# The first 64 rows of the last two experts in one shared fp32 tile ahead of the expert loop

## The chip, the cores and the metric

The kernel runs on one core of one Trainium2 chip. What counts is device time in microseconds (us), from the start to the end of one launch.

## The reference

Three stages follow each other. Attention with a mask that keeps the 32 largest scores of each row (4 batches, 8 heads, 576 rows, head size 64) gives x of 2304 x 512. A dense layer with a squared ReLU, `(relu(x @ w_in)**2) @ w_out` with 2048 hidden columns, gives the next x. Then each row goes to one of eight experts, or to none:

```python
do_compute = x @ w_skip > 0
out = x.copy()
xc = x[do_compute]
logits = xc @ w_gate
e_idx = np.argmax(logits, axis=1)
gate_w = softmax(logits)[np.arange(len(xc)), e_idx]
for e in range(8):
    mask = e_idx == e
    h = np.maximum(xc[mask] @ w1[e], 0.0)      # w1[e]: 512 x 1024
    y[mask] = gate_w[mask, None] * (h @ w2[e]) # w2[e]: 1024 x 512
out[do_compute] = xc + y
```

With the inputs used here 921 of the 2304 rows are kept: 244, 93, 269, 118, 84, 48, 48 and 17 for experts 0 to 7.

## The kernel before

All engines run one written-out program each, and semaphores order them. The first 750 us are the attention and the dense layer, interleaved in a loop over time steps `t` (to `TIMES`); TensorE is busy nearly without a gap. The rows of x are worked in nine groups of 256 (`ORDER`); the last group's two column blocks are called late, the sixteen before it early.

The router is worked out by VectorE in many short dependent operations on tiles of 2 to 18 columns per partition (`link` makes each wait for the one before it): which expert each row has (`pick_experts`), its gate (`set_gates`), its rank within its expert (`my_rank`), how many 128-row tiles each expert needs (`ntiles`) and where they begin (`tile_from`), and from these the tile (`my_tile`) and place of each row. TensorE turns this into a table of row numbers by 18 small matmuls (L1565); from it VectorE sets `gather_tab` (L1240), and GpSimd gathers the rows of a tile from `rows_gated` in DRAM by an indirect DMA (L739).

To cover this wait, one tile is worked ahead: the first 128 early rows of expert 0 (`ahead_rows`, `ahead_w1`, `ahead_w2`), in plain fp32 with the raw weights. Its up matmuls (`up_ahead`, L1481), its transposes (`transpose_ahead`) and its down matmuls (L1586) are placed among the table's steps on TensorE. Six of the eight down matmuls come before the transposes of tile 0's rows (`transpose_rows(0)`, L1573), which wait for the gather, and two after.

The expert loop then runs over tiles `s`, each with one expert, in the order of experts. Each tile is computed to nearly fp32 accuracy from fp32r products of high and low parts: ScalarE writes the high part of each weight piece (`w1_high` L966, `w2_high` L972), VectorE and GpSimd the low part (`w1_low` L1267, `w2_low` L1273 and L735), and TensorE multiplies high by high, low by high and high by low (L1600, L1605, L1609 up; L1631, L1636, L1639 down). The w1 pieces of tile `s + 1` are split in the second half of tile `s`; two of VectorE's four are made before the result `yo` of tile `s` (L1300), which GpSimd scatters to `out` (L763). The first four tiles always run, the rest under `If(tiles > s)`.

Raw weights lie in `weights`, three slots of 32 KB per partition (w1 in the first half, w2 in the second). The loop uses slots 0 and 1 in turn by the expert's number; slot 2 is the place of `w1_high` and `w2_high`. Before, slots 1 and 2 held the split `w_in` of the dense layer. SyncE loads each expert in four pieces of 1 MB (`load_expert`, L474), two outstanding; an expert's load starts when the splits of the expert two before it are done. All eight experts are loaded whatever the counts, and SyncE waits for all of them at the end, reads four registers and waits for the scatters. Which slot and which load a tile needs is read from `meta` into registers; past the last tile the tables name expert 7.

Of the kernel before, what the change touches and what calls it, by code (L numbers as in the profile page):

```python
# [52 lines left out]
def build(nc, qT, kT, v_main, v_tail, w_in, w_out, w9, w1, w2, rows_scratch, out):  # L53
# [74 lines left out]
    MIDDLE = N // 2  # L128
    E = NE
# [10 lines left out]
    with ExitStack() as ctx:  # L140
# [53 lines left out]
        with (nc.sbuf_tensor("values", [P, NCOL, 2, SLOTS], F16) as values,  # L194
              nc.sbuf_tensor("ahead_rows", [P, D + 4], F32) as ahead_rows, nc.sbuf_tensor("ahead_xT", [P, D], F32) as ahead_xT,
              nc.sbuf_tensor("ahead_values", [P, EARLY, 2], F16) as ahead_values):
            pass
# [118 lines left out]
        ahead_stored = sem("ahead_stored")  # L316
        places_set = sem("places_set")
# [26 lines left out]
        ahead_w2 = weights[:, 0, KC * F2:WCOL].rearrange("p (f n) -> p f n", f=F2T)  # L344
        xg = tail[:, 3 * F2:3 * F2 + DEEP * (D + 4)].rearrange("p (b n) -> p b n", b=DEEP)
# [22 lines left out]
        expert, parity, empty = (temp(SLOTS) for _ in range(3))  # L368
        ahead = temp(EARLY)
# [63 lines left out]
        def _(sp):  # L433
# [48 lines left out]

            load_kq(0)
# [13 lines left out]
            for t in range(TIMES):  # L497
# [43 lines left out]
                for j in range(GROUPS):  # L541
                    if ENDS[j] != t:
                        continue
                    sp.wait_ge(rows_copied, 2 * j + (2 if j < GROUPS - 1 else 1))
# [13 lines left out]

            for e in range(1, E):
                if e == 1:  # L560

                    sp.wait_ge(unit_up, NU)
# [7 lines left out]
                for n in range(4):  # L570
# [3 lines left out]
                    if e >= RING and n == 2:  # L574

                        wait_apart(sp, w2_low_v, 3 * first + 1)
                        wait_apart(sp, w2_low_p, first + 1)
                    if e == 1 and n == 2:

                        sp.wait_ge(gates_set, 2)  # L580
                        store_gates(ORDER[-1][0] * S + ORDER[-1][1] * W, [EARLY, EARLY + 1])
                    load_expert(e, n)
            for par in range(2):
                sp.wait_ge(expert_loaded[par], 2 * E * LOADS)
            sp.wait_ge(ahead_stored, 16)
            turns = [sp.value_load(meta[0:1, x:x + 1], min_val=1, max_val=TURNS)
# [5 lines left out]
        def _(pool):  # L592
# [144 lines left out]
            def gather(s):  # L737
# [5 lines left out]

            gather(0)
# [10 lines left out]
                in_=yo[:, DEEP - 1, :], in_offset=None, bounds_check=N - 1, oob_is_err=False).then_inc(ahead_stored, 16)  # L755

# [20 lines left out]
        def _(act):  # L777
# [173 lines left out]
            exponentiate_logits(EARLY, 2)  # L951
            rectify_ahead(0)
            rectify_ahead(1)
            copy_ahead(0)
            copy_ahead(1)
            act.wait_ge(meta_set, 1)
# [24 lines left out]
            def routed_tile(s):  # L981
# [4 lines left out]
                wait(act, down_done, s)  # L986
                split_w2_high(at, (3, 0, 1))
                place[:] = [expert_at(act, s + 1), expert_need(act, s + 1)]
                act.wait_ge(up_done, 2 * s + 1)
                if s == 0:  # L990

                    act.wait_ge(ahead_down, 1)
# [173 lines left out]


# [521 lines left out]
```

## Time and profile before

| | us |
|---|---|
| median of 3 runs | 924.42 (924.35 to 924.54) |
| the profiled execution | 924.49 |
| its span, first to last instruction | 922.7 |
| TensorE (PE) busy in it | 883.8 |
| VectorE (DVE) busy | 819.3 |
| ScalarE (ACT) busy | 658.5 |
| GpSimd (POOL) busy | 656.9 |

The span is counted from the first instruction; some 1.8 us of the execution lie around it. Times in the rows below are from the span's start. Busy shares are means over stages that differ; the change acts on the last 170 us, so those have to be read by themselves.

### The profile page before, as it was taken

The numbers are of one execution on the slowest core, as the hardware profiler recorded it, in microseconds if no ns is written. First come the engines' busy times: TensorE is split into PE (matmuls) and PEld (weight loads), VectorE is DVE, ScalarE is ACT, GpSimd is POOL, SyncE is SP. The second block draws the span as 40 slices with busy tenths as digits, with TensorE's granted clock in tenths as the row PEclk, the third lists the DMA queues.
The fourth block names the chain that finished last, engine by engine and source line by source line (L and its number), as shares of the span: only waits on it lengthen the run. The fifth ranks groups of instructions, "written<-read, shape, count | busy, mean of one in ns | idle before, by whom it ended". The sixth has DMA issues, their size and how long they took to land.

```text
span 922.7 us, 21066 instructions
## 1 busy us (share of the span) xinstructions
PE 883.8 (96%) x6674; PEld 716.9 (78%) x6674; DVE 819.3 (89%) x2584; ACT 658.5 (71%) x1297; POOL 656.9 (71%) x884
## 2 busy tenths in 40 slices
PE   3799899999999999999999999999999999999997
PEld 1677688887888878888788887888878886788886
DVE  5999999999999999999999999999992064888887
ACT  2778787777777778777777777877775322788886
POOL 1899998877877887787787788778777552444432
PEclk9999999999999999999999999999999999999999
DMA  8963543466343658956545455543533775764990
GB/s 307 361 235 97 185 142 124 139 213 195 134 165 129 207 185 273 257 177 231 167 141 164 136 178 178 175 124 118 187 122 117 243 249 203 266 235 149 348 336 10
DMA packets 69750, 175.40 MB, mean 190 GB/s; under 512 B 21298, under 2 KB 26418, under 8 KB 65280
## 3 DMA queue, kind: packets, MB, share of 16 engines
q1 hardware_dynamic: 67792, 168.91, 54.8%
q0 software_dynamic: 1840, 5.06, 1.8%
q8 instruction: 56, 0.92, 0.4%
q14 instruction: 62, 0.51, 0.2%
HBM read 154.19 MB, written 21.27 MB: 190 GB/s over the span
## 4 chain that ended last, share of the span: by engine, by line
PE 84%; DVE 11%; POOL 2%; issue 1%; ACT 1%; DMA 0%; SPq 0%; DVEq 0%; POOLq 0%
PE psum L1334 8%; PE psum L1399 7%; PE psum L1400 7%; PE psum L1401 7%; PE psum L1359 7%; PE psum L1416 7%; PE psum L1417 7%; PE psum L1378 7%; PE psum L1418 7%; DVE top L1036 3%; DVE upper L1041 3%; PE psum L1631 2%; PE psum L1600 2%; PE psum L1605 2%; PE psum L1636 2%; PE psum L1639 2%
## 5 line engine op out<-in xcount | busy, mean ns | idle before, releaser
L1036 DVE MAX8 top<-upper 128x8 f32<-128x288 f32 x576 | 239.0, 446 | 0.0
L620 POOL TENSOR_TENSOR s_sb<-s_sb,below 128x576 f32<-128x576 f32 x144 | 203.3, 1433 | 1.5 <-ACT below L792 1.5
L1041 DVE MATCH_REPLACE8 upper<-top,upper 128x288 f32<-128x288 f32 x432 | 187.7, 441 | 0.0
L1399 PE MATMUL psum<-x_high,w_in_high 128*128 128x256 f32 x576 | 168.2, 292 | 1.6 <-POOL x_low L626 1.1
L783 ACT ACTIVATE s_sb<-psum 128x576 f32<-128x576 f32 x144 | 93.8, 651 | 96.9 <-PE psum L1334 87.4
L1400 PE MATMUL psum<-x_low,w_in_high 128*128 128x256 f32 x576 | 161.8, 281 | 0.0
L1401 PE MATMUL psum<-x_high,w_in_low 128*128 128x256 f32 x576 | 161.2, 280 | 0.0
L635 POOL TENSOR_TENSOR square<-relu 128x256 f32<-128x256 f32 x144 | 89.6, 622 | 81.6 <-ACT relu L825 80.9
L640 POOL TENSOR_TENSOR g_low<-square,g_high 128x256 fp32r<-128x256 f32 x144 | 108.4, 753 | 30.2 <-POOL square L635 23.0
L1334 PE MATMUL psum<-k_sb,q_sb 64*128 64x288 f32 x512 | 101.3, 473 | 26.8 <-DVE lower L1027 18.6
L792 ACT ACTIVATE below<-s_sb,steep_kth 128x576 f32<-128x576 f32 x144 | 110.8, 770 | 9.3 <-POOL neg_max L608 8.4
L1051 DVE MAX8 top<-lower 128x8 f32<-128x288 f32 x288 | 115.4, 441 | 0.0
L1416 PE MATMUL psum<-w_ring,g_high 128*128 128x512 f32 x288 | 114.5, 398 | 0.0
L1417 PE MATMUL psum<-w_ring,g_high 128*128 128x512 f32 x288 | 113.5, 394 | 0.0
L1418 PE MATMUL psum<-w_ring,g_low 128*128 128x512 f32 x288 | 113.2, 393 | 0.0
L1399 PEld LDWEIGHTS psum<-x_high,w_in_high 128*128 128x128 f32 x576 | 108.5, 188 | 6.0 <-POOL x_low L626 1.3
L1400 PEld LDWEIGHTS psum<-x_low,w_in_high 128*128 128x128 f32 x576 | 108.7, 189 | 3.2
L800 ACT ACTIVATE s_sb<-s_sb,neg_max 128x576 f32<-128x576 f32 x144 | 110.9, 770 | 0.0
L825 ACT ACTIVATE relu<-psum 128x256 f32<-128x256 f32 x144 | 55.5, 385 | 76.1 <-PE psum L1401 75.0
L1401 PEld LDWEIGHTS psum<-x_high,w_in_low 128*128 128x128 f32 x576 | 108.6, 189 | 0.0
L614 POOL TENSOR_SCALAR s_sb<-s_sb,sums 128x576 f32<-128x576 f32 x144 | 106.2, 748 | 0.0
L1359 PEld LDWEIGHTS psum<-ident,s_sb 128*128 128x128 f32 x576 | 62.1, 142 | 34.0 <-issue 30.2
(213 smaller groups left out, 1844.0 us busy)
## 6 DMA issues: line engine op xcount, KB each, us to landing
w_ring<-w_split SPq DMA_DIRECT2D x144, 512.0 KB, 4.6
weights<-w SPq DMA_DIRECT2D x32, 1024.0 KB, 7.3
v_sb<-v_main SPq DMA_DIRECT2D x48, 256.0 KB, 2.6
w_split<-w_ring SPq DMA_DIRECT2D x16, 512.0 KB, 3.9
k_sb<-kT SPq DMA_DIRECT2D x32, 144.0 KB, 4.6
k_sb<-kT SPq DMA_DIRECT2D x32, 128.0 KB, 4.4
q_sb<-qT SPq DMA_DIRECT2D x32, 128.0 KB, 4.0
weights<-w_out SPq DMA_DIRECT2D x1, 4096.0 KB, 14.1
```

The source lines that it names most:

```text
L620: nc.gpsimd.tensor_tensor(s_sb[:, s % SBUFS, n, 0:S], s_sb[:, s % SBUFS, n, 0:S], below[:, n, :], ALU.subtract).then_inc(masked, 1)
L1036: v.max(top[:, s % 2, n, 8 * r:8 * r + 8], upper[:, s % 2, n, :]).then_inc(upper_step, 1)
L1041: v.match_replace(upper[:, s % 2, n, :], top[:, s % 2, n, 8 * r:8 * r + 8], upper[:, s % 2, n, :], LOWEST).then_inc(upper_step, 1)
L1051: v.max(top[:, s % 2, n, at:at + 8], lower[:, s % 2, n, :]).then_inc(lower_step, 1)
L1334: last = t_.matmul(psum[:, n, 0:HALF], q_sb[own, a % RING_A, r * P:(r + 1) * P], k_sb[own, a % RING_A, cols], start=True, stop=True)
L1359: t_.transpose(psum[:, 2 + n, k * P:(k + 1) * P], tiles[:, at:at + P], ident[:, :])
L1399: t_.matmul(dst, wh, x_high[:, j % 2, k, :], start=k == 0, stop=False)
L1400: t_.matmul(dst, wh, x_low[:, j % 2, k, :], start=False, stop=False)
L1401: last = t_.matmul(dst, wl, x_high[:, j % 2, k, :], start=False, stop=k == KC - 1)
L1416: t_.matmul(psum[:, 6 + c, :], gh, wh, start=f == 0, stop=False)
L1417: t_.matmul(psum[:, 6 + c, :], gh, wl, start=False, stop=False)
L1418: last = t_.matmul(psum[:, 6 + c, :], gl, wh, start=False, stop=f == FT - 1)
```

## The change

A second tile is worked between the tile ahead and the expert loop, in plain fp32 with raw weights. Its upper 64 rows are the first 64 rows of expert 7, its lower 64 those of expert 6. Each expert's matmuls use half of TensorE's columns: the stationary operand is 128 x 64, the output goes to 64 of PSUM's partitions. The two halves alternate matmul by matmul.

- SyncE loads the pair's four 2 MB halves: expert 7's w1 to slot 2 when the dense layer's up matmuls are done, expert 6's w1 to slot 1 after the last row stores, both w2 once `gather_tab` is set. Expert 1's own load, which stood there, comes after: its w1 after `pair_up`, its w2 after `pair_down`.
- ScalarE's DMA queue stores the late rows' gates in place of SyncE's.
- VectorE takes the 64 rows out of the ranks and counts of experts 6 and 7 (`share_tile`, called twice; three operations for `ntiles` in place of two; two more for `my_tile`) and gives them tile number `PAIR` in the table. It works `yo` of the tile ahead before, not after, the w1 pieces of tile 0, and `x_low` of tile 0 after all four of them.
- GpSimd gathers the pair's rows before tile 0's, and scatters the pair's result after the tile ahead's.
- TensorE transposes the pair's rows where it transposed tile 0's, and after `ahead_down` does the pair's up matmuls, the transposes of its hidden rows (tile 0's rows between them) and its down matmuls, then the loop.
- ScalarE copies and rectifies for the pair ahead of `split_w1_high` of tile 0, and splits tile 0's w2 after `pair_down`.

```diff
@@ -342,6 +358,12 @@
...
+        pair_at = [RING, 1]
+        pair_w1 = [weights[:, at, 0:KC * F2].rearrange("p (k f) -> p k f", k=KC) for at in pair_at]
+        pair_w2 = [weights[:, at, KC * F2:WCOL].rearrange("p (f n) -> p f n", f=F2T) for at in pair_at]
+        pair_xT, pair_hT = ahead_xT, ahead_hT
@@ -479,6 +502,12 @@
...
+            def load_pair(x, part):
+                sp.dma_start(weights[:, pair_at[x], part * KC * F2:(part + 1) * KC * F2], (w1, w2)[part][E - 1 - x, :, :]
+                             ).then_inc(pair_loaded[part], 16)
@@ -541,6 +570,10 @@
...
+                    if j == GROUPS - 1:
+                        sp.wait_ge(unit_up, NU)
+                        load_pair(0, 0)
@@ -556,10 +589,14 @@
...
+            sp.wait_ge(rows_stored[(GROUPS - 1) % 2], STORED[GROUPS - 1])
+            load_pair(1, 0)
+            sp.wait_ge(table_set, 1)
+            load_pair(0, 1)
+            load_pair(1, 1)
...
-                if e == 1:
-                    sp.wait_ge(unit_up, NU)
@@ -575,14 +612,19 @@
                         wait_apart(sp, w2_low_p, first + 1)
+                    if e == 1 and n == 0:
+                        sp.wait_ge(pair_up, 2)
                     if e == 1 and n == 2:
-                        sp.wait_ge(gates_set, 2)
-                        store_gates(ORDER[-1][0] * S + ORDER[-1][1] * W, [EARLY, EARLY + 1])
+                        sp.wait_ge(pair_down, 1)
...
                 sp.wait_ge(expert_loaded[par], 2 * E * LOADS)
+            for part in range(2):
+                sp.wait_ge(pair_loaded[part], 2 * 16)
             sp.wait_ge(ahead_stored, 16)
+            sp.wait_ge(pair_stored, 16)
@@ -741,6 +783,9 @@
...
+            nc.gpsimd.indirect_dma_start(
+                out=pair_rows[:, :], out_offset=None, in_=rows_gated[:, :],
+                in_offset=bass.IndirectOffsetOnAxis(ap=gather_tab[:, PAIR:PAIR + 1], axis=0)).then_inc(pair_gathered, 16)
@@ -753,6 +798,10 @@
...
+            pool.wait_ge(pair_y_done, 1)
+            nc.gpsimd.indirect_dma_start(
+                out=out[:, :], out_offset=bass.IndirectOffsetOnAxis(ap=scatter_tab[:, PAIR:PAIR + 1], axis=0),
+                in_=yo[:, DEEP - 2, :], in_offset=None, bounds_check=N - 1, oob_is_err=False).then_inc(pair_stored, 16)
@@ -949,10 +998,25 @@
...
+            act.wait_ge(gates_set, 2)
+            first = ORDER[-1][0] * S + ORDER[-1][1] * W
+            act.dma_start(rows_gated[first:first + W, D:D + 4].rearrange("(c p) n -> p c n", p=P), gate4[:, EARLY:NCOL, :]
+                          ).then_inc(gates_stored, 16)
...
+            act.wait_ge(pair_turned, 1)
+            nc.scalar.activation(pair_xT[:, :], psum[:, 4, :], ACT.Copy).then_inc(pair_xT_done, 1)
+            for half in range(2):
+                act.wait_ge(pair_up, half + 1)
+                nc.scalar.activation(h_sb[:, half * 512:(half + 1) * 512], psum[:, half, :], ACT.Relu).then_inc(pair_h_done, 1)
+            for half in range(2):
+                act.wait_ge(pair_hT_done, half + 1)
+                nc.scalar.activation(pair_hT[:, half * 512:(half + 1) * 512], psum[:, 2 + half, :], ACT.Copy
+                                     ).then_inc(pair_hT_copied, 1)
@@ -984,12 +1048,12 @@
                 wait(act, down_done, s)
+                if s == 0:
+                    act.wait_ge(pair_down, 1)
...
                 act.wait_ge(up_done, 2 * s + 1)
-                if s == 0:
-                    act.wait_ge(ahead_down, 1)
@@ -1164,6 +1228,19 @@
...
+            def share_tile(cols):
+                link(v.tensor_tensor(in_pair[:, cols], onehot[:, cols, E - 2], onehot[:, cols, E - 1], ALU.add))
+                link(v.scalar_tensor_tensor(out=my_rank[:, cols], in0=in_pair[:, cols], scalar=-float(SHARE),
+                                            in1=my_rank[:, cols], op0=ALU.mult, op1=ALU.add))
+                link(v.scalar_tensor_tensor(out=paired[:, cols], in0=my_rank[:, cols], scalar=0.0, in1=in_pair[:, cols],
+                                            op0=ALU.is_lt, op1=ALU.mult))
+                link(v.scalar_tensor_tensor(out=pair_shift[:, cols], in0=onehot[:, cols, E - 1], scalar=-float(SHARE),
+                                            in1=paired[:, cols], op0=ALU.mult, op1=ALU.mult))
+                link(v.tensor_tensor(far[:, cols], far[:, cols], pair_shift[:, cols], ALU.add))
@@ -1217,17 +1295,23 @@
...
             dve.wait_ge(ranks_done, 2)
-            count_tiles(ntiles, counts_psum, 63.5)
+            link(v.tensor_scalar(ntiles, counts_psum, 63.5, 1.0 / P, ALU.add, ALU.mult))
+            link(v.tensor_scalar(ntiles[:, E - 2:E], ntiles[:, E - 2:E], -SHARE / P, None, ALU.add))
+            link(v.tensor_scalar(ntiles, ntiles, MAGIC, -MAGIC, ALU.add, ALU.add))
...
             link(v.tensor_reduce(out=my_rank[:, late], in_=hit[:, late, :], axis=AX_X, op=ALU.add))
+            share_tile(late)
...
             link(v.tensor_tensor(my_tile, my_tile, over, ALU.add))
+            link(v.scalar_tensor_tensor(out=my_tile, in0=paired, scalar=1.0, in1=my_tile, op0=ALU.is_lt, op1=ALU.mult))
+            link(v.scalar_tensor_tensor(out=my_tile, in0=paired, scalar=float(PAIR), in1=my_tile, op0=ALU.mult, op1=ALU.add))
@@ -1302,16 +1388,19 @@
                 split_w1_low(s + 1, place[0], 3)
-            split_w1_low(0, place[0], 0)
-            split_w1_low(0, place[0], 1)
-            split_x_low(0)
-            split_w1_low(0, place[0], 2)
-            split_w1_low(0, place[0], 3)
...
                                    in1=ahead_rows[:, 0:D], op0=ALU.mult, op1=ALU.add).then_inc(ahead_y_done, 1)
+            for n in range(4):
+                split_w1_low(0, place[0], n)
+            split_x_low(0)
+            dve.wait_ge(pair_down, 1)
+            dve.wait_ge(pair_gathered, 16)
+            v.scalar_tensor_tensor(out=yo[:, DEEP - 2, :], in0=psum[:, 6, :], scalar=pair_rows[:, D:D + 1],
+                                   in1=pair_rows[:, 0:D], op0=ALU.mult, op1=ALU.add).then_inc(pair_y_done, 1)
@@ -1582,11 +1671,43 @@
                 if f == F2T - 2:
-                    transpose_rows(0)
+                    pe.wait_ge(pair_gathered, 16)
+                    for k in range(KC):
+                        last = t_.transpose(psum[:, 4, k * P:(k + 1) * P], pair_rows[:, k * P:(k + 1) * P], ident[:, :])
+                    last.then_inc(pair_turned, 1)
...
             last.then_inc(ahead_down, 1)
+            pe.wait_ge(pair_xT_done, 1)
+            pe.wait_ge(pair_loaded[0], 2 * 16)
+            for half in range(2):
+                for k in range(KC):
+                    for x in range(2):
+                        to = slice(x * SHARE, (x + 1) * SHARE)
+                        last = t_.matmul(psum[to, half, :], pair_xT[:, k * P + x * SHARE:k * P + (x + 1) * SHARE],
+                                         pair_w1[x][:, k, half * 512:(half + 1) * 512], start=k == 0, stop=k == KC - 1)
+                last.then_inc(pair_up, 1)
...
             tiles = tiles_in_all(pe)
+            for half in range(2):
+                if half == 1:
+                    transpose_rows(0)
+                pe.wait_ge(pair_h_done, half + 1)
+                for k in range(4):
+                    at = half * 512 + k * P
+                    last = t_.transpose(psum[:, 2 + half, k * P:(k + 1) * P], h_sb[:, at:at + P], ident[:, :])
+                last.then_inc(pair_hT_done, 1)
+            pe.wait_ge(pair_loaded[1], 2 * 16)
+            for f in range(F2T):
+                if f % 4 == 0:
+                    pe.wait_ge(pair_hT_copied, f // 4 + 1)
+                for x in range(2):
+                    to = slice(x * SHARE, (x + 1) * SHARE)
+                    last = t_.matmul(psum[to, 6, :], pair_hT[:, f * P + x * SHARE:f * P + (x + 1) * SHARE],
+                                     pair_w2[x][:, f, :], start=f == 0, stop=f == F2T - 1)
+            last.then_inc(pair_down, 1)
```

## Rows read from the trace of the kernel before

**Rows 1.** The page, part 1: busy time, share of the span, instructions.

```profile
PE 883.8 (96%) x6674; PEld 716.9 (78%) x6674; DVE 819.3 (89%) x2584; ACT 658.5 (71%) x1297; POOL 656.9 (71%) x884
```

**Rows 2.** The chain that ended last: start us, us, what; around tiles 0 and 9.

```profile
789.63 1.72 PE psum L1586 x4
791.35 0.93 PE psum L1600 x4
...
796.93 0.44 PE psum L1618 x4
...
798.27 1.02 PE psum L1631 x4
...
904.63 0.93 PE psum L1600 x4
```

**Rows 3.** Timeline of VectorE: start us, us, engine, line, operation, output and input.

```profile
777.46 0.15 DVE L1154 TENSOR_SCALAR s_sb<-psum 128x8 f32<-128x8 f32 x1
...
779.07 0.31 DVE L1228 TENSOR_TENSOR s_sb<-onehot,s_sb 128x144 f32<-128x144 f16 x1
...
783.00 0.19 DVE L1240 TENSOR_SCALAR gather_tab<-psum 128x32 uint32<-128x32 f32 x1
```

**Rows 4.** Timeline of TensorE's weight loads, 782 to 789 us; in brackets idle before.

```profile
782.30 0.11 PEld L1565 LDWEIGHTS psum<-values,place_hit 128*128 128x128 f16 x2 [0.21 <-DVE place_hit L1164]
...
788.81 0.58 PEld L1573 LDWEIGHTS psum<-ident,tail 128*128 128x128 f32 x4 [0.44 <-DMA tail<-rows_gated,gather_tab]
```

**Rows 5.** Timeline of GpSimd: the first gather.

```profile
783.99 0.99 POOL L739 DMA_INDIRECT tail<-rows_gated,gather_tab  x1 [15.75 <-DVE gather_tab L1240]
```

**Rows 6.** The line of the gathers (L739): duration ns and landing, min/median/max.

```profile
L739 POOL DMA_INDIRECT tail<-rows_gated,gather_tab x11: 949/1941/1947, 784.0 to 882.5; - x11
...
DMA to landing us min/median/max: 3.6/6.0/8.8
```

**Rows 7.** DMA issues of 857 to 858 us: count, us to landing.

```profile
tail<-rows_gated,gather_tab POOLq DMA_INDIRECT x1, 7.2
```

**Rows 8.** Busy us of PE, PEld, DVE, ACT, POOL, granted clock, DMA share, GB/s.

```profile
784.00:786.00 2.00, 2.00 (x5) 0.83 (x5) 1.72 (x11) 0.00 (x0) 0.98 (x1) 1.00 0.98 401
786.00:788.00 2.00, 2.00 (x6) 0.95 (x5) 0.52 (x2) 1.86 (x2) 0.18 (x1) 1.00 0.53 216
```

**Rows 9.** Timeline of TensorE, 305 to 307 us: matmuls in column halves.

```profile
305.94 1.09 PE L1378 MATMUL psum<-pT_sb,v_sb 128*64 128x128 f32 x16
306.87 0.39 PE L1378 MATMUL psum<-pT_sb,v_last 128*64 128x128 f32 x4
```

**Rows 10.** The line of these matmuls (L1378): weight loads, ns min/median/max.

```profile
L1378 PEld LDWEIGHTS psum<-pT_sb,v_sb x1024: 132/137/137, 40.0 to 716.6; 128*64 128x64 f32 x171
```

**Rows 11.** Busy and granted clock (the 0.72) after the last matmul.

```profile
919.00:920.00 1.00, 0.00 (x0) 0.00 (x0) 1.00 (x2) 0.00 (x0) 1.00 (x1) 0.72 0.03 8
```

**Rows 12.** Timeline of TensorE at the start of its dense work.

```profile
32.18 1.97 PE L1359 MATMUL psum<-ident,s_sb 128*128 128x128 f32 x8 [0.22 <-POOL s_sb L614]
...
34.16 5.22 PE L1475 MATMUL psum<-ident 128*128 128x128 f32 x40
```

**Rows 13.** Timeline of SyncE's queue: the last load of an expert.

```profile
894.89 0.33 SPq L474 DMA_DIRECT2D weights<-w  x1
```

**Rows 14.** Timeline of all engines in the last tile.

```profile
912.58 3.90 ACT L966 ACTIVATE w_high<-weights 128x1024 fp32r x4
...
913.78 2.77 DVE L1267 TENSOR_TENSOR w_low<-weights,w_high 128x1024 fp32r<-128x1024 f32 x2 [0.25 <-ACT w_high L966]
...
917.25 0.75 DVE L1300 SCALAR_TENSOR_TENSOR yo<-psum,tail 128x512 f32<-128x512 f32 x1 [0.71 <-PE psum L1639]
...
918.86 1.14 POOL L763 DMA_INDIRECT out<-yo,scatter_tab  x1 [4.54 <-DVE yo L1300]
```

**Rows 15.** Waits of SyncE's queue, 900 to 923 us: us in total, times, longest.

```profile
SPq L50 <- DMA out<-yo,scatter_tab: 18.6, 2, 12.3
SPq L585 <- DMA weights<-w: 5.2, 1, 5.2
```

More of the change, by code:

```diff
@@ L128, in build @@
     MIDDLE = N // 2
+    SHARE = P // 2
+    PAIR = SLOTS - 1
+    assert PAIR > MOST + 1
     E = NE
@@ L195, in build @@
               nc.sbuf_tensor("ahead_rows", [P, D + 4], F32) as ahead_rows, nc.sbuf_tensor("ahead_xT", [P, D], F32) as ahead_xT,
-              nc.sbuf_tensor("ahead_values", [P, EARLY, 2], F16) as ahead_values):
+              nc.sbuf_tensor("ahead_values", [P, EARLY, 2], F16) as ahead_values,
+              nc.sbuf_tensor("pair_rows", [P, D + 4], F32) as pair_rows):
             pass
@@ L316, in build @@
         ahead_stored = sem("ahead_stored")
+        pair_loaded = [sem("pair_loaded0"), sem("pair_loaded1")]
+        pair_gathered = sem("pair_gathered")
+        pair_turned = sem("pair_turned")
+        pair_xT_done = sem("pair_xT_done")
+        pair_up = sem("pair_up")
+        pair_h_done = sem("pair_h_done")
+        pair_hT_done = sem("pair_hT_done")
+        pair_hT_copied = sem("pair_hT_copied")
+        pair_down = sem("pair_down")
+        pair_y_done = sem("pair_y_done")
+        pair_stored = sem("pair_stored")
         places_set = sem("places_set")
@@ L368, in build @@
         expert, parity, empty = (temp(SLOTS) for _ in range(3))
+        in_pair, paired, pair_shift = (temp(NCOL) for _ in range(3))
         ahead = temp(EARLY)
@@ L1198, in _ @@
             v.tensor_copy(early_sum[:, :, :], early_total.unsqueeze(1).to_broadcast([P, 2, E])).then_inc(early_sum_set, 1)
+            share_tile(slice(0, EARLY))
             count_tiles(over[:, 0:EARLY], ranks, -63.5)
@@ L1297, in routed_tile @@
                 wait(dve, y_stored[x], 16 * (s // DEEP))
+                if s == DEEP - 2:
+                    dve.wait_ge(pair_stored, 16)
                 if s == DEEP - 1:
@@ L1627, in routed_tile @@
                         wait(pe, y_done, s - 1)
+                        if s == 0:
+                            pe.wait_ge(pair_y_done, 1)
                         if s == 1:
```

## The prediction

> **What bounds the kernel now.** I read the page first: TensorE is busy for 96% of the span [rows 1]. Then the chain of waits over the end of the run, because the change touches nothing before about 757 us. The routed tiles follow each other with no gap: the first up matmul of the first one starts at 791.35 and that of the tenth at 904.63 [rows 2], so a tile costs (904.63 - 791.35) / 9 = 12.59 us of TensorE. Ten tiles is what the reference's arrays give: 921 rows are kept, 244, 93, 269, 118, 84, 48, 48 and 17 for experts 0 to 7, and after the 128 rows of expert 0 that go ahead the experts need 1, 1, 3, 1, 1, 1, 1, 1 tiles. Ahead of the loop the path is different: VectorE's short routing operations, then the table of rows, then the gather. In the changed kernel the shared tile takes up to 64 rows of each of experts 6 and 7, which is all of their 48 and 17, so both of their tiles vanish and tile 7, expert 5's, becomes the last.
>
> **Removed: two tiles**, 2 x 12.59 = 25.2 us, all on TensorE's path.
>
> **Added on VectorE.** Eight short operations enter the late chain ahead of the table: one for the tile counts, five of share_tile, two for my_tile. The eight links from 777.46 to 779.07 take 1.61 us, 0.20 each [rows 3]. TensorE already waits for the end of this chain (place_hit, 0.21 us) [rows 4], so the 1.6 us are paid in full: the gather table, set by the operation at 783.00, and the down matmuls of the tile ahead both slip by 1.6. The same five operations on the early columns fall ahead of a stretch in which VectorE idles and cost nothing.
>
> **Added: a gather on the path.** Now the gather of tile 0 is issued at 783.99 and TensorE, having done six of the eight down matmuls, waits 0.44 us for it until 788.81 [rows 4, 5]. Then transposes and two matmuls are left, 2.4 us to tile 0 [rows 2]. The pair's gather takes exactly this place and starts at 785.6; without a stall it would be wanted at 788.4 + 1.6 = about 790.2. What differs is the traffic: before, only the rest of expert 1's load is in flight, and the DMA share falls to 0.53 by 787 [rows 8]; after, SyncE issues two loads of 2 MB each on the same event, 0.7 us ahead of the gather, so it travels under full load. The gathers range from 3.6 us to 8.8 us, with 6.0 in the middle, and one inside the loop, under loads, took 7.2 [rows 6, 7]. Its issue took 1.94 us there against 0.95 in the open, so 6 to 8 us stand for a loaded gather with 8 KB rows; the pair's rows are 16 KB, which could double what it waits for them (8.8 - 1.0 - 3.6 = 4.2, doubled 8.4, plus 3.6: 12). Bounds: 4.8, as the first gather had it (no stall), and 12 (a stall of 7). I take 8.3, a little over the loaded rows: it lands at 793.9, a stall of 3.7 against 790.2, of which 0.1 to 0.4 was there before; 3.6 us.
> The Trainium skill (DMA: Bandwidth & Descriptors, Queues, rings and completion order) says that each DMA engine takes turns between its queues at the granularity of a packet. The trace agrees so far as loaded gathers take longer; what the rule would make of a 16 KB row is rival (d).
>
> **Added: the pair itself.** Up and down are 16 matmuls each of 128 x 64 weights by 512 columns, in two passes each: 64 records. A full-width record of 512 columns takes 1.72 / 4 = 0.43 us [rows 2]. Whether two halves run at once is the largest term. The trace has the form, at 128 columns: L1378 alternates halves in the same order, and 16 records start over 306.87 - 305.94 = 0.93 us, 0.058 each [rows 9], where full width would need 0.43 / 4 = 0.108. So two halves overlap, at 0.54 of the full time. By that ratio the 64 records take 64 x 0.43 x 0.54 = 14.9 us; if the 0.004 us above the half is a price for each record, 64 x (0.215 + 0.004) = 14.0; I take 14.4 (bounds 13.8, wholly overlapped, and 27.5, not at all). The eight transposes of the hidden rows, with tile 0's four between them, last as in a tile, 798.27 - 796.93 = 1.3 us [rows 2], with ScalarE's copies in the same order as there. ScalarE's four w1 pieces of tile 0 can't come earlier than behind pair_up, since w1_high lies over the pair's w1 in slot 2; with some 1.5 us of register loads and 3.9 us [rows 14] behind its copies they fit under the pair's down matmuls (7.2 us). VectorE now makes xT_low behind all four w1_low pieces, about 0.3 us after tile 0 wants it. Sum 14.4 + 1.3 + 0.3 = 16.0.
> GpSimd issues the pair's gather ahead of tile 0's, which slips by 1 us and is wanted 7 us later; it waits for pair_y_done ahead of route_tile(0), 1.5 us into tile 0, whose first need of GpSimd is the w2 piece 7 us in. ScalarE's store of the gates holds back its relu of the tile ahead by about 1 us, and the transposes that want it stand behind eight more records, 3.4 us.
> The Trainium skill (TensorE: Matmul & The Clock Gate, Part 3) says that weight loads overlap matmuls in flight only where the row group differs, which halves of the columns don't satisfy. The trace speaks against it for this form: L1378's weight loads take 137 ns each [rows 10] and its records come every 58.
>
> **Weights.** The w2 of the pair, 4.2 MB at the 401 GB/s of a full stretch [rows 8], needs 10.5 us plus some 2.5 from 785, with the gathers about 800; it is wanted when the hidden rows are copied, at 791.35 + 1.6 + 3.6 + 7.2 + 1.3 = 805. It costs nothing; if slower by half it costs up to 1. The second w1, issued behind the row stores, has from 777 to 794. Expert 1's loads move from SyncE's place ahead of the loop to behind pair_up and pair_down; they are wanted 8 and 12 us into tile 0 and are 2 MB each: hidden.
>
> **Clock.** TensorE would idle for 3.6 us. At the end of the trace the granted clock falls inside 919 to 920 (mean 0.72, so at 919.4), 2.2 us after the last matmul, at about 917.2 [rows 11, 14]; at the start it was low from 32.18, where a transpose takes 0.22 to 0.25 us, into the 40 keep_clock records, whose mean is 5.22 / 40 = 0.13 against 0.11 at full clock [rows 12]: some 3 us at the lower level (1.2 GHz of 2.4), so 1.5 us lost. Bounds 0 (no fall) and 3; I take 1.2.
>
> **The tail, where a wait appears.** ScalarE splits w1 of tile s + 1 in tile s whether or not there is such a tile; VectorE makes two low pieces of it before the result yo. For tile 8 the tables name expert 7, which has no tile now, but whose load is waited for. SyncE's last 1 MB loads are issued one by one as those before them land: the last at 894.89, when the second w1 piece of expert 7 lands [rows 13]. Tile 7 starts at 879.43 = 904.63 - 2 x 12.60, so that is 15.5 us into tile 7; before, tile 8 used it at 900. After, two gathers of some 1 us each are missing from this stretch (those for tiles 9 and 10) and 15.5 becomes 13 (bounds 11.5 and 15.5). From there: ScalarE's start at 912.58, two low pieces done at 913.78 + 2.77, yo, and the scatter's issue 1.6 us behind yo's start: about 912.58 to 918.2, 5.6 us with the idle 0.7 taken out [rows 14]. Scatter's landing and the end follow as now, 922.7 - 918.86 = 3.8. So the run ends 13 + 5.6 + 3.8 = 22.4 us after tile 7's start, against 922.7 - 904.63 = 18.1 for the last tile now: 4.3 us. SyncE's own end is close: the last load lands about 19 us in, the four register loads take some 2.5 (it waited until 900.4 for the last load and then 18.6 us for two scatters, of which the 12.3 end at 921.5) [rows 15]. Bounds: 2 (loads early) and 7.
>
> **Sum** against the profiled 924.5 (span 922.7 + 1.8; the median is 0.07 lower): 924.5 - 25.2 + 1.6 + 3.6 + 16.0 + 1.2 + 4.3 = 926.0. The saving is real, but the pair eats two thirds of it and waits the rest.
>
> **Rivals.** (a) The gather lands in time and the clock holds: 926.0 - 4.8 = 921.2. For it: the first gather's 4.8 us under a load; against: two doubled loads issued ahead of it. 0.17. (b) The tail is free, because expert 7's w1 lands by 8 us into tile 7: 921.7. Against it stand the issue times above. 0.12. (c) Slower: the halves don't overlap at 512 columns. Then the pair costs 27.5 instead of 14.4: 939.1. It decides from 0.29 us a record on, where the pair costs some 4 us more and 926.0 becomes 930. Against: L1378. 0.07. (d) The gather waits behind a whole 16 KB row at each turn: the upper end of 12 us, 3.7 later than taken, 929.7; the pair's w2 coming late, or a clock low through the pair, end at about 930 too. For it: the spread from 3.6 to 8.8 with rows of half the size. 0.10. The Trainium skill's rule of turns by packets (same page and section) is this one. (e) That no tile goes away: the counts, and the ten tiles of the trace, exclude it nearly.
>
> **From these to the numbers.** The forecast, with its own range of 923 to 930, has 0.54; 0.2% (1.85 us) is what a measurement here tells from no change, so it is split by 926.3: 0.28 same, 0.26 slower. Faster: all of (a), 0.07 of (b): 0.24. Same: 0.28 + 0.05 = 0.33. Slower: 0.26 + 0.17 = 0.43. The range leaves out (c) and the ends of (a) and (d): 919.5 to 932.
>
> **What would show it.** Eight L1639 groups of eight instead of ten; L1378's pace in the pair's lines (0.22 us a record); the wait of the pair's transposes on the gather, 3 to 4 us; a stretch with clock under 1 after it; tile 0 starting at 813.7; VectorE waiting in the last tile on ScalarE's w1 piece, and it on the DMA. The prediction is wrong if the gather lands within 5 us or the last tile ends like the others.

## The result: 0.44% slower, and the profile after

| | us |
|---|---|
| changed kernel, median of 11 runs | 928.02 (924.66 to 932.01) |
| kernel before, 11 runs beside it | 924.32 (923.98 to 924.57) |
| ratio | 1.0044 [1.0034, 1.0055] |
| profiled execution of the changed kernel | 930.86, span 929.1 |

Forecast were 926.0, a range of 919.5 to 932, and slower as the likeliest of the three. The runs of the changed kernel now spread over 7 us, those of before over 0.6. The profiled one is one of the longer ones (+6.4 against the profile before, +3.7 between the medians); the accounting below is made within the profiles, and the spread is itself one of the findings.

The page, parts 1 and 3 (answers to [rows 1]: PE had 883.8 us and 96%):

```profile
PE 877.4 (94%) x6630; PEld 702.8 (76%) x6630; DVE 800.1 (86%) x2576; ACT 640.8 (69%) x1276; POOL 645.6 (69%) x880
...
q10 hardware_dynamic: 272, 0.00, 0.0%
```

TensorE does 6.4 us less work and the run is longer: it waits more. The second line is ScalarE's DMA queue, the small store of the gates that the change put there.

The chain that ended last, from the gates to tile 0 (start us, us, what); it answers [rows 2], where tile 0 began at 791.35:

```profile
777.35 8.37 DMA rows_gated<-gate
...
786.57 9.57 DMA pair_rows<-rows_gated,gather_tab
...
796.19 1.12 PE psum L1677 x4
797.30 2.60 PE psum L1679 x4
799.91 7.02 PE psum L1689 x32
806.93 0.59 PE psum L1700 x4
807.51 0.44 PE psum L1662 x4
807.95 0.44 PE psum L1700 x4
808.39 7.02 PE psum L1708 x32
815.40 1.13 PE psum L1721 x4
```

L1677 are the pair's transposes, L1679 the last down matmuls of the tile ahead, L1689 the pair's up and L1708 its down matmuls, L1721 is tile 0. Ahead of them stand two DMAs, not an engine. The timeline of TensorE and of GpSimd (start, us, line, operation; in brackets the idle time before and what ended it) answers [rows 4, 5]:

```profile
785.19 7.08 PE L1679 MATMUL psum<-weights,tail 128*128 128x512 f32 x12 [0.78 <-ACT tail L997]
796.19 1.12 PE L1677 MATMUL psum<-ident,pair_rows 128*128 128x128 f32 x4 [3.92 <-DMA pair_rows<-rows_gated,gather_tab]
...
786.57 0.99 POOL L786 DMA_INDIRECT pair_rows<-rows_gated,gather_tab  x1 [18.55 <-DMA rows_gated<-gate]
```

Busy time of PE, PEld, DVE, ACT, POOL, then the granted clock, the DMA share and GB/s, by stretches of 2 us; the first two answer [rows 8], where the clock was 1.00 in both:

```profile
784.00:786.00 2.00, 1.22 (x5) 0.57 (x4) 1.83 (x8) 0.60 (x1) 0.00 (x0) 0.83 0.50 99
786.00:788.00 2.00, 2.00 (x4) 0.90 (x3) 1.28 (x8) 0.00 (x0) 1.13 (x2) 0.50 0.72 262
788.00:790.00 2.00, 2.00 (x5) 0.77 (x5) 0.00 (x0) 0.00 (x0) 1.56 (x2) 0.82 0.98 418
...
796.00:798.00 2.00, 1.81 (x6) 1.30 (x7) 0.00 (x0) 0.60 (x1) 0.00 (x0) 0.50 1.00 414
798.00:800.00 2.00, 2.00 (x6) 0.72 (x6) 0.06 (x1) 0.00 (x0) 0.00 (x0) 0.76 0.92 376
```

And the last tile, which began at 903.56: the chain (start us, us, what), and below it the timeline of VectorE, whose yo answers that of [rows 14] at 917.25:

```profile
904.92 8.27 DMA weights<-w
...
913.21 5.90 DMA weights<-w
...
919.28 1.06 ACT w_high L1030
...
920.47 0.90 DVE w_low L1351
```

```profile
922.75 0.75 DVE L1386 SCALAR_TENSOR_TENSOR yo<-psum,tail 128x512 f32<-128x512 f32 x1
```

The second piece of expert 7's w1 is issued at 913.21 and lands at 919.11, 15.5 us into the tile; ScalarE splits it for a tile that doesn't exist, VectorE makes two low pieces of it, and only then the result that everything else was ready for. The run ends 25.5 us after the start of its last tile, against 18.1.

This is a queue of loads, not one slow load. SyncE's timeline, before and after, where the sixteen pieces of experts 4 to 7 begin:

```profile
844.84 0.83 SPq L474 DMA_DIRECT2D weights<-w  x2
```

```profile
869.17 0.82 SPq L497 DMA_DIRECT2D weights<-w  x2
```

That is 53.5 and 53.8 us after tile 0, and from there they follow each other nearly without a pause, each piece issued as one before it lands. Expert 7's second w1 piece lands 103.5 us after tile 0 before (894.89, [rows 13]) and 103.7 after. The loads have not slowed down; the last tile now begins 88.2 us after tile 0, and before it was 113.3.

The account of the two profiles: tile 0 later by 24.05, two tiles gone (-25.2), tail longer by 7.4: +6.3 of the +6.4.

### The profile page after: what moved, and what is told of

The parts are those of the page before. It is cut to its first block, busy times and chain, and to the rows that moved or that the text cites. A ratio compares the mean times of both kernels' runs of the same rounds, so it can differ in the third digit from the quotient of the medians.

```text
span 929.1 us, 20865 instructions
## 1 busy us (share of the span) xinstructions
PE 877.4 (94%) x6630; PEld 702.8 (76%) x6630; DVE 800.1 (86%) x2576; ACT 640.8 (69%) x1276; POOL 645.6 (69%) x880
## 4 chain that ended last, share of the span: by engine, by line
PE 76%; DVE 11%; DMA 8%; POOL 2%; issue 1%; ACT 1%; SPq 0%; DVEq 0%; POOLq 0%; ACTq 0%
PE psum L1423 8%; PE psum L1488 7%; PE psum L1489 7%; PE psum L1490 7%; PE psum L1448 7%; PE psum L1505 7%; PE psum L1506 7%; PE psum L1467 7%; PE psum L1507 7%; DMA weights<-w 5%; DVE top L1100 3%; DVE upper L1105 3%; DVE top L1115 1%; PE psum L1470 1%; PE psum L1429 1%
## 5 line engine op out<-in xcount | busy, mean ns | idle before, releaser
L682 POOL TENSOR_TENSOR g_low<-square,g_high 128x256 fp32r<-128x256 f32 x144 | 106.1, 737 | 30.5 <-POOL square L677 23.2
L1507 PE MATMUL psum<-w_ring,g_low 128*128 128x512 f32 x288 | 113.3, 393 | 0.0
```

Source lines behind the costliest of these rows:

```text
L1507: last = t_.matmul(psum[:, 6 + c, :], gl, wh, start=False, stop=f == FT - 1)
```

## The experiments

Each is the changed kernel with the edit shown. The kernel before gave medians of 924.62 beside e1 to e4, 924.79 beside e5 to e8 and 924.20 beside e9 and e10, and the ratios are against those.

**e1_no_tail_load: the last tile without the useless load.**

```diff
-            for e in range(1, E):
+            for e in range(1, E - 2):
...
+            link(v.tensor_scalar(expert, expert, float(E - 3), None, ALU.min))
```

> Experts 6 and 7, which have no tile of their own with these inputs, are not loaded in the loop (8 MB less), and the tables name expert 5 for the tile behind the last. Theory (the last tile waits for a load that nobody uses): the last tile ends 18.1 us after its start, as before the change, in place of 25.4; the time falls by 5 to 7.5 us, to about 921 to 923, and the spread between runs shrinks to a few tenths of a us. Rival (the end is late because SyncE reads its registers late, or the traffic slows the tiles): under 2 us are gained, 926 to 928, and the spread stays.

Measured: 925.91 (925.10 to 927.39), ratio 1.0014 [1.0005, 1.0023]. The last tile again waits for TensorE, and ends 18.9 us after its start:

```profile
917.00 0.75 DVE L1387 SCALAR_TENSOR_TENSOR yo<-psum,tail 128x512 f32<-128x512 f32 x1 [1.05 <-PE psum L1763]
```

The mechanism is shown, but its size is not the one expected: 5 to 7.5 us were, and between the medians it is 2.1 (2.4, when each is taken against the kernel before beside it). The 7.4 us of the account belong to one of the longer runs. In the other profiles that keep the load, ScalarE's split of it started 11.8 (e2), 12.1 (e6), 12.9 (e5), 14.2 (e4), 15.5 (e9) and 15.6 us (e3) into the last tile, always late, by a varying amount. Without it the runs spread over 2.3 us in place of 7.3, not over the few tenths expected. Ahead of the loop nothing was gained: here TensorE waited 6.0 us for the pair's gather. TensorE's timeline shows why the wait is longer than the 3.9 of the changed kernel:

```profile
782.93 0.96 PE L1655 MATMUL psum<-values,place_hit 128*128 128x64 f16 x18 [1.92 <-DVE values L1316]
...
785.16 5.39 PE L1680 MATMUL psum<-weights,tail 128*128 128x512 f32 x12 [0.78 <-ACT tail L997]
```

It stood idle for the same 1.9 and 0.8 us as in the changed kernel, yet the clock stayed at 1.00 and the twelve records took 5.39 us in place of 7.08, so TensorE came to its wait 1.7 us sooner.

**e2_gather_first: the pair's w2 waits for the gather.**

```diff
-            sp.wait_ge(table_set, 1)
+            sp.wait_ge(pair_gathered, 16)
             load_pair(0, 1)
```

> The pair's two w2 loads wait for the pair's gather to land, not for the table. Theory (the gather is late since it shares the DMA engines with 4 MB): it lands in 3.7 to 5 us in place of 9.6, TensorE's wait for it falls from 3.9 us to under 0.5, the granted clock stays at 1.00 between 792 and 800; the w2 weights then land about 803, where they are wanted about 801, so 2 to 3 us are given back there: 924.5 to 926.5 in place of 928.0. Rival (the gather is slow by itself, as it reads rows whose stores are recent): it still takes over 8 us and the kernel becomes slower by 6 us or more, since w2 comes later still.

Measured: 929.98 (927.49 to 931.15), ratio 1.0061 [1.0047, 1.0074]. The chain:

```profile
786.79 3.72 DMA pair_rows<-rows_gated,gather_tab
```

The timeline of TensorE:

```profile
805.96 9.44 PE L1708 MATMUL psum<-weights,tail 128*64 128x512 f32 x32 [4.54 <-DMA weights<-w]
```

Alone on the queues the gather takes 3.7 us and TensorE doesn't wait for it; the load beside it is what made it 9.6. But w2 is now issued 6 us later, at 790.9 in place of 785.0 for the second of its loads, and its 4.2 MB land at 805.9. With its stall gone TensorE wants them at 801.4, waits 4.5 us and does the down matmuls partly at the lower clock (9.44 against 7.02), and tile 0 starts at 815.40, as without the edit. The prediction had w2 there by 800, wanted at 805: a slack of 5 us, and the delay is 6. The wait only moved; the 1.5 to 3.5 us expected from the edit did not come.

**e3_halves_in_turn: all matmuls of one half, then of the other.**

```diff
-                for k in range(KC):
-                    for x in range(2):
+                for x in range(2):
+                    for k in range(KC):
```

and the same for the down matmuls.

> The same 32 matmuls of the pair, but all of one half of the columns before all of the other (in each bank of the up stage, and in the down stage). Theory (neighbours in different halves run at once): records come every 0.43 us in place of 0.22, up and down take 13.8 us each in place of 7.0, and the run takes 13 to 14 us more. Rival (the pace of 0.22 us is a property of 64-column matmuls and needs no neighbour): no change in the pace and the time.

Measured: one run, 939.13, so the time has no spread to be read against and the reading is of the trace. The two groups in the chain:

```profile
801.08 8.90 PE psum L1689 x32
...
811.43 12.22 PE psum L1708 x32
```

In turn the 64 records take 21.1 us, alternating 14.0: the halves do run at the same time. Expected were 13 to 14 us more, measured are 7.1, since 64 x 0.43 would be 27.5. The up part changes halves three times and takes 8.90 / 0.43 = 20.7 records' time, 11.3 less than 32; the down part changes once and takes 28.4, 3.6 less. So by these two sums each change of half hides nearly four records. The Trainium skill (TensorE: Matmul & The Clock Gate, Part 3) has weight loads overlap matmuls in flight only where the row group differs; the alternating halves show otherwise, with weight loads of 137 ns each and a record every 219 ns, half the time of a half alone.

**e4_keep_clock: unread small matmuls where TensorE idles** (8 behind the first transposes of the tile ahead and ahead of the table, 24 ahead of the wait for the gather; added work that nobody reads).

```diff
...
             transpose_ahead(0)
+            keep_clock(8, 3)
...
+                    keep_clock(24, 3)
                     pe.wait_ge(pair_gathered, 16)
```

> Eight small matmuls that nobody reads fill TensorE's idle time ahead of the table, 24 more the one ahead of the pair's gather. Theory (TensorE's idle time lowers the granted clock, which costs 1.6 us behind the gather): the clock reads 1.00 throughout from 776 to 816, the four transposes take 0.44 us in place of 1.1 and the two matmuls behind them 1.7 in place of 2.6; 926.4 in place of 928.0. Rival (the lower clock is hidden by the waits): under 0.5 us.

Measured: 927.18 (926.43 to 928.62), ratio 1.0028 [1.0017, 1.0038].

```profile
786.00:788.00 2.00, 2.00 (x6) 0.84 (x5) 1.30 (x9) 0.00 (x0) 0.99 (x1) 1.00 0.60 188
...
796.00:798.00 2.00, 2.00 (x9) 0.86 (x6) 0.00 (x0) 0.60 (x1) 0.00 (x0) 1.00 0.94 373
```

The clock stays at 1.00 where it was 0.50, and from the pair's transposes to its up matmuls it is 0.44 + 1.72 us in place of 1.12 + 2.60: 1.56 us, the price of the second fall. The first (786 to 788) only made TensorE reach its wait later. That the eight matmuls are what prevented it is not shown: in e1, e2 and e3 the clock stayed at 1.00 there without them. The 24 have a price of their own. The gather took 8.0 us here and landed at 794.7, and they ended at 796.02, so 1.3 us were lost again. Between the medians, each against the kernel before beside it, the gain is 1.1 us, and the intervals of the two ratios overlap at their edge.

**e5_w2_pieces: the pair's w2 in rows of 4 KB.** The same bytes on the same event, each load in four DMAs.

```diff
+                for c in range(4):
+                    sp.dma_start(weights[:, pair_at[x], part * KC * F2 + c * size:part * KC * F2 + (c + 1) * size],
+                                 (w1, w2)[part][E - 1 - x, :, c * size:(c + 1) * size]).then_inc(pair_loaded[part], 16)
...
```

> The pair's two w2 loads are cut into four loads each, with 4 KB per partition in place of 16 KB; bytes, place and event stay. Theory (at each turn of a DMA engine the gather waits for a whole row of the loads): the gather, issued at the same time, lands in 5 to 6.5 us in place of 9.6, TensorE's wait for it falls from 3.9 to 6 us to about 1, the low clock behind it goes too, and the run is 3 to 5 us shorter at the end of the pair's up stage; w2 lands about as before. Rival (the gather waits for all bytes queued ahead of it, whatever the rows): it lands after 9 us or more again, and nothing moves.

Measured: 927.71 (922.99 to 931.78), ratio 1.0035 [1.0017, 1.0052], by the time alone not to be told from the changed kernel; its profile is the second fastest of the ten runs.

**e6_all_pieces: expert 6's w1, in flight beside the gates' store, cut in the same way too.**

> As e5, and expert 6's w1 load for the pair, which runs beside the late gates' store, cut in the same way. Theory of turns by rows: the gates' store lands in 5 to 6 us in place of 8.4, and the pair's gather is issued 1 us earlier, at 785.5; another 0.5 to 1 us beyond e5. Rival: the store still takes over 8 us and e6 equals e5.

Measured: 924.35 (922.54 to 927.00), ratio 0.9995 [0.9985, 1.0006]. The chains of e5 and of e6:

```profile
777.23 8.51 DMA rows_gated<-gate
...
786.59 7.18 DMA pair_rows<-rows_gated,gather_tab
```

```profile
785.55 7.34 DMA pair_rows<-rows_gated,gather_tab
```

The cut of w2 brings the gather from 9.6 to 7.2 us and TensorE's wait from 3.9 to 1.8; the clock doesn't fall behind that wait, and tile 0 starts at 811.7. With w1 cut too the gates' store takes 5.4 us in place of 8.4 and is no longer on the chain: the gather is issued behind its table, 1.0 earlier, TensorE waits 0.5, and tile 0 starts at 810.8, 4.6 earlier than in the changed kernel. The lengths of the two small transfers follow the row length of the large ones beside them, whose bytes are the same. Eight small loads are also issued over a longer time than two large ones, so less is queued ahead of the gather; the trace's packet records say that this is not it. The gather's first packet moves 4.2 us after its issue with either row length (790.78 and 790.85; without load 1.7), and the engines are busy with the load until then in both. From the first packet to the landing it is 5.4 us beside packets of 16 KB, which take 0.61 us each, and 2.9 beside packets of 4 KB, which take 0.16. So the rows of 16 KB in place of 4 explain 2.4 of the 5.9 us that the load costs the gather, and 2.5 come ahead of the first packet whatever the rows. This is the mechanism of rival (d), at a smaller size (9.6 us, not 12). By the Trainium skill (DMA: Bandwidth & Descriptors, Queues, rings and completion order) queues take turns packet by packet; the two runs agree with that.

The cut has a price: w2 lands at 799.6 in the changed kernel and at 803.5 with the cuts (e10), 4 us later. Here it is wanted at 803.3 or after.

**e9_down_first: the wait for the gather behind all eight down matmuls of the tile ahead.**

```diff
-                if f == F2T - 2:
-                    pe.wait_ge(pair_gathered, 16)
-                    for k in range(KC):
...
             last.then_inc(ahead_down, 1)
+            pe.wait_ge(pair_gathered, 16)
+            for k in range(KC):
```

> The changed kernel with one thing altered: the four transposes of the pair's rows, and TensorE's wait for the pair's gather in front of them, move behind the last two down matmuls of the tile ahead (1.7 us, four records) instead of in front. Theory, that TensorE's stall is a wait for a gather whose landing does not depend on TensorE: the gather lands at about 796.2 again, the wait shrinks from 3.9 to 2.2 us, but ScalarE's copy of the turned rows, which the two matmuls used to cover, now stands open, 0.6 to 0.9 us, so tile 0 starts 0.8 us earlier, at 814.6, and the time is 927.2. Rival, that the pair's w2 is what is late, hidden behind the gather: the pair's down matmuls wait for it and tile 0 stays at 815.4, the time at 928.0.

Measured: 928.35 (925.82 to 930.75), ratio 1.0038 [1.0020, 1.0056], nothing that can be told from the changed kernel. The waits of TensorE (us, times, longest), then the chain:

```profile
PE psum L1678 <- DMA pair_rows<-rows_gated,gather_tab: 1.4, 1, 1.4
...
PE psum L1688 <- ACT ahead_xT L1011: 0.7, 1, 0.7
```

```profile
798.46 8.65 PE psum L1688 x32
```

The wait for the gather fell to 1.4 (expected 2.2; the lower clock also reached further into the down matmuls this time), but the copy stands open, and the second stretch of lower clock, which lay on the transposes and the last down matmuls before (3.72 us for 2.16), now lies on the up matmuls, 8.65 in place of 7.02. From the gather's landing to tile 0 it is 18.5 in place of 19.3 us; the store and the chain ahead of it happened to be 0.9 later in this profile, so tile 0 came at 815.59. w2 was not waited for, so the rival falls, but the gain is too small for the medians to confirm.

**e10_pieces_tail: the cuts of e6 and the edit of e1 together.**

> The changed kernel with two things altered together: the pair's loads cut into rows of 4 KB (expert 7's w1, which has nobody near it, stays whole), and no load of experts 6 and 7 in the loop, whose tiles don't exist (that part of the weights traffic is left out). If the stall ahead of the loop and the tail are two separate losses that add up, tile 0 starts at about 811 as with the cuts alone and the last tile ends 19 us after its start as without the loads alone: 924.35 - (22.7 - 18.9) = 920.6. The rest to the 918.6 of the kernel with the extra matmuls and the other order is then the clock and the order on TensorE. Rival, that the two are coupled through the DMA queues (the loads of the loop start earlier when tile 0 does, and land earlier in the last tile anyway): the gain beyond the cuts alone is under 2 us, 922.5 or more.

Measured: 919.85 (919.45 to 920.51), ratio 0.9954 [0.9940, 0.9967]. The two losses are separate: beyond the cuts alone (e6) it gains 3.9 us, each against the kernel before beside it, where 3.8 were expected and the rival had under 2. Tile 0 starts at 810.59, the last tile ends 18.9 after its start. The gains of e6 and e1 over the changed kernel (4.1 and 2.4) sum to 6.5 of e10's 8.0; the changed kernel's spread of 7 us leaves that difference open. TensorE's waits:

```profile
PE psum L1683 <- ACT tail L1000: 0.8, 1, 0.8
PE psum L1681 <- DMA pair_rows<-rows_gated,gather_tab: 0.2, 1, 0.2
PE psum L1712 <- DMA weights<-w: 0.2, 1, 0.2
```

Of the waits ahead of the loop these are left. The last is new: with the gather out of the way, the pair's w2, cut in pieces, is just late (the last piece issued at 788.43, landed at 803.46).

**e7_together: as e10, with w2 issued without the wait for the table, the order of e9, and the 8 matmuls of e4.**

```diff
-            sp.wait_ge(table_set, 1)
             load_pair(0, 1)
...
+            keep_clock(8, 3)
```

> The cuts of e6, the w2 loads issued at once behind the w1 load without waiting for the table, all eight down matmuls of the tile ahead in front of the wait for the pair's gather, eight unread small matmuls ahead of the table, and experts 6 and 7 not loaded in the loop, as in e1 (they have no tile of their own with these inputs). Theory (the pair's own work costs 15.5 us and everything above it is waiting): tile 0 starts at about 808.5 in place of 815.4, the last tile ends 18 to 19 us after its start, and the run takes 917 to 919.5 us, below both kernels. Rival (DMA supply ahead of the loop is the bound whatever the order): tile 0 starts at 812 or later, and the run takes 922 or more.

Measured: 918.61 (918.22 to 919.31), ratio 0.9933 [0.9919, 0.9946].

```profile
784.00:786.00 2.00, 1.22 (x8) 0.77 (x9) 1.79 (x8) 0.60 (x1) 0.39 (x1) 1.00 1.00 354
786.00:788.00 2.00, 2.00 (x6) 0.88 (x5) 1.72 (x10) 0.00 (x0) 1.55 (x2) 1.00 1.04 397
```

The queues are full from 784 on (0.50 and 0.72 in the changed kernel), the clock holds, and tile 0 starts at 809.52, 1.1 us before e10's. Three things were altered against e10 at once, so their shares are not shown.

**e8_general: e7 with loads that depend on the counts.** e1, e7 and e10 leave out the loads of experts 6 and 7 because these inputs need none. Here SyncE reads a flag and skips an expert without a tile.

```diff
+            link(v.tensor_scalar(meta_f[:, 2 * SLOTS + E + DEEP + 1:], ntiles, 0.5, None, ALU.is_gt))
...
+                    used_at_all = sp.value_load(meta[0:1, at:at + 1], min_val=0, max_val=1)
+                    with sp.If(used_at_all > 0):
...
+                    with sp.If(used_at_all < 1):
+                        for par in range(2):
+                            sp.wait_ge(expert_loaded[par], 2 * e * LOADS)
+                            sp.sem_inc(expert_loaded[par], 2 * LOADS)
```

> As e7, but without knowing the counts: VectorE writes a flag for each expert that has a tile, and SyncE loads an expert under that flag, or else adds to the loads' semaphores what the loads would have added. Theory (only the traffic and the wait of the last tile matter): as e7 within 1 us, 917 to 920.5. Rival (two more register reads and a branch for each expert delay the loads so that a tile waits): 1 to 4 us slower than e7.

Measured: 918.59 (918.27 to 919.97), ratio 0.9935 [0.9921, 0.9948]. The flag costs nothing that shows, and this version beats the kernel before by 6.2 us and the changed one by about 10.

## Why the prediction was right and wrong

- Two tiles: 25.2 us, as forecast; from tile 0 to the last tile it is (903.56 - 815.40) / 7 = 12.59 us a tile again.
- VectorE's eight links: gather_tab set 1.6 us later relative to the dense stage's end, as forecast. What the step missed is that TensorE then idles for 1.9 us in place of 0.3 and is busy 1.22 of the two us from 784 instead of 2.00 [rows 8], after which its clock may fall to 0.50: of the eight profiles with this gap unfilled it fell in five (the changed kernel, e5, e6, e9, e10) and stayed in three (e1, e2, e3). What decides between them is open.
- The gather: taken 8.3 us, measured 9.6, between the nearest rows and rival (d), which doubled the whole wait of 4.2 us beside 8 KB rows; e5 and the packet records show that only a part of the wait goes with the rows. A term was missing ahead of it: the gates' store, moved to another queue, was costed by what it holds back on ScalarE and not by its own landing beside 16 KB rows. It took 8.4 us and became what the gather waits for, +1.0. Together the gather landed 2.3 us later than in the sum.
- The stall of TensorE was 3.9 against 3.7, right by chance: the clock's first fall made TensorE late for its own wait by 1.7 us. Where it didn't fall and the rest was the same (e1, e3), the stall was 6.0.
- The pair: 16.0 forecast, 15.5 measured (799.91 to 815.40). The 64 records take 14.04 us, 0.219 each, the lower of the two ratios drawn from L1378; ScalarE's pieces and x_low cost nothing that shows. Rival (c) is excluded by e3.
- The clock behind the stall: 1.2 forecast, 1.56 measured (e4).
- Together these account, within half a us, for tile 0 at 815.4 instead of 813.7.
- The weights: not waited for, right, but the slack was small: e2 spends it by issuing them 6 us later, and e10, which wants them earlier and gets them later, meets it.
- The tail is the term that was mis-sized most: 4.3 forecast, 7.4 in the profile. The landing of expert 7's second w1 piece was put at 13 us into the tile and came at 15.5, the upper bound given. That 15.5 was the row of before; the 2.5 us taken off it, for two gathers that are missing from the stretch, had no row behind them, and in this profile nothing came off. The end after the scatter's issue was 4.8 and not 3.8. The mechanism is shown by e1. Over the profiles the start of the split ranges from 11.8 to 15.7 us, so the median's tail is probably nearer to the forecast, which no profile of a median run shows: the changed kernel's median is 2.0 above the forecast, its profile 4.9.
- Rivals (a) and (b) named the right two places. e6 is (a) made true but for the clock, 924.35 in place of 921.2: in its profile (923.49) the tail is 22.7 (22.4 in the forecast), and tile 0 at 810.8 stands 1.9 later than in (a), of which the clock's first fall is 1.7; e10 is both together, and with these two waits gone the pair is worth 0.46%.

What stays open: why the last landing varies by 4 us. In the seven profiles that keep the loads, the first piece of expert 6 is issued 79.3 to 80.6 us after tile 0, and expert 7's second w1 piece lands 99.8 to 103.7 after it, so nearly all of the spread arises in the last six loads. With gathers and scatters on the same queues, no run here isolates it further.

## What to carry to other kernels

When a change takes work off the critical engine, list the transfers that are still issued for that work, and who waits for them: a load for a tile that no longer exists cost 7.4 us in the profiled run here and made the runs spread. Of a small transfer that is on the path, a part is priced by the row length of what flows beside it, so cut the large loads into short rows, where they can land some 4 us later, rather than delay them; delaying them (e2) only moved the wait. And after each wait look at the granted clock, since a pause of TensorE can be paid twice.

## What the runs showed of the hardware

- Beside loads of 16 KB per partition row, a gather of 128 rows took 9.4 to 9.6 us (8.0 in e4) and the gates' store (16 bytes a row) 8.4 to 8.9; beside the same bytes in 4 KB rows the gather took 6.8 to 7.3 (e5 to e8, e10) and the store 5.1 to 5.4 (e6 to e8, e10); with nothing beside it the gather took 3.7.
- Under either kind of load the gather's first packet moved 4.2 us after the issue (changed kernel and e5), without load after 1.7 (e2). A 16 KB packet took 0.61 us, a 4 KB one 0.16.
- From 788 to 800, in stretches of 2 us with the queues full, e6 moved 331 to 420 GB/s and the changed kernel 353 to 425. The pair's w2 in 4 KB rows landed at 803.5 (e10), in 16 KB rows at 799.6.
- Matmuls of 128 x 64 weights by 512 fp32 columns in alternating halves of the output partitions come at 0.219 us a record, half of the 0.43 of one half alone. When one half's run ends and the other's begins, about 3.7 records of the new one are already hidden behind the old, an estimate from e3's two groups.
- The granted clock is not settled by the length of TensorE's pauses alone. Behind idle times of 1.9 and 0.8 us, with short matmuls between, it fell to 0.50 in five profiles and stayed at 1.00 in three; with eight unread matmuls in the first of these gaps it stayed in all three (e4, e7, e8). Before tile 0 it fell behind 6.0 us (e1), 4.5 us (e2) and 3.9 us (changed kernel), and behind 1.4 and then 0.7 us (e9), but not behind 1.8 us (e5).
